# Bucketed attention with two gated layers: epsilon summed as a second column, two exponents in a burst step, normalisation behind the burst

## The reference, cut to what matters

```python
batch, n_heads, seq, head_dim = 2, 8, 768, 64
q_bits = (einsum('bhsd,dk->bhsk', q, proj) > 0)        # 6 bits, the same for k
mask = q_bucket[:, :, :, None] == k_bucket[:, :, None, :]
scores = where(mask, scale * q @ k.T, -1e9)
attn = exp(scores - max(scores))
attn = attn / (sum(attn, axis=-1) + 1e-09)
x = (attn @ v)  as (B, S, H * D)
gate = sigmoid(causal 5-tap convolution of x, per channel)
x = (gate * (x @ w_val)) @ w_out
xk, xr = x mixed with the row before it by mu_k, mu_r
out = sigmoid(xr @ w_r) * (relu(xk @ w_k) ** 2 @ w_v)
```

## Time and profile before

| | |
|---|---|
| median of 3 runs | 528.86 us (528.14 to 529.12) |
| the profiled execution's own time | 530.34 us |
| its span, first to last instruction | 528.5 us |
| TensorE matmul busy | 479.9 us, 91% |
| VectorE busy | 355.8 us, 67% |
| ScalarE busy | 281.0 us, 53% |
| GpSimd busy | 271.9 us, 51% |
| mean granted TensorE clock | 0.99 |

### The profile page before, as it was taken

How to read it: one execution, slowest core, us unless ns; L and a number is a source line. 1 busy time by engine, 2 the same in 40 slices (tenths; PEclk the granted TensorE clock), 3 DMA queues, 4 the chain that set the end, 5 groups by cost and what they waited for, 6 DMA issues and landing times.

```text
span 528.5 us, 9376 instructions
## 1 busy us (share of the span) xinstructions
PE 479.9 (91%) x3504; PEld 406.6 (77%) x3504; DVE 355.8 (67%) x603; ACT 281.0 (53%) x601; POOL 271.9 (51%) x259
## 2 busy tenths in 40 slices
PE   2879889898797888987999999999999999999997
PEld 1656666565565665665666999899999999999997
DVE  2676677976877869768785788778478578534211
ACT  3686775767558665776656453345245245144140
POOL 5592653826617458165505654646446446444240
PEclk9999999999899998999999999999999999999999
DMA  5021030210212102101013100100100100100101
GB/s 190 30 81 47 2 125 15 96 45 2 96 44 93 34 16 95 45 23 44 17 25 115 36 2 1 42 1 1 41 1 1 42 1 1 42 1 1 41 2 40
DMA packets 10574, 20.81 MB, mean 39 GB/s; under 512 B 1696, under 2 KB 6816, under 8 KB 10528
## 3 DMA queue, kind: packets, MB, share of 16 engines
q1 hardware_dynamic: 10224, 19.94, 11.5%
q10 hardware_dynamic: 304, 0.27, 0.2%
HBM read 17.06 MB, written 3.15 MB: 38 GB/s over the span
## 4 chain that ended last, share of the span: by engine, by line
PE 69%; DVE 15%; issue 8%; ACT 7%; DMA 1%; POOL 0%; ACTq 0%; DVEq 0%
PE ps L670 25%; PE ps L678 11%; PE ps L658 11%; PE ps L620 10%; PE ps L634 8%; DVE gate L828 3%; ACT q L434 2%; ACT probs L442 2%; DVE sums_e L805 2%; DVE negmax L786 2%; PE ps L644 1%; PE ps L595 1%; DVE pt L793 1%; DVE k L778 1%; DVE tmp_a L897 1%
## 5 line engine op out<-in xcount | busy, mean ns | idle before, releaser
L786 DVE TENSOR_REDUCE negmax<-ps 128x1 f32<-128x768 f32 x96 | 91.8, 956 | 62.9 <-PE ps L620 62.2
L620 PE MATMUL ps<-k,q 128*128 128x384 f32 x384 | 96.1, 374 | 20.5 <-ACT probs L442 18.4
L620 PEld LDWEIGHTS ps<-k,q 128*128 128x128 f32 x384 | 66.2, 197 | 37.4 <-issue 28.0
L634 PE MATMUL ps<-ident,probs 128*128 128x128 f32 x576 | 84.6, 282 | 10.8 <-DVE pt L793 10.3
L442 ACT ACTIVATE probs<-ps,negmax 128x768 f32<-128x768 f32 x96 | 86.5, 901 | 12.6 <-DVE negmax L786 10.6
L634 PEld LDWEIGHTS ps<-ident,probs 128*128 128x128 f32 x576 | 70.0, 145 | 19.9 <-DVE pt L793 11.5
L658 PE MATMUL ps<-pt,vals 128*64 128x384 f32 x384 | 70.2, 502 | 2.7 <-DVE x L818 2.7
L450 ACT ACTIVATE pt<-ps 128x384 f32<-128x384 f32 x96 | 46.7, 487 | 34.4 <-PE ps L634 33.1
L400 POOL TENSOR_TENSOR h_lo<-tmp_b,h_hi 128x256 fp32r<-128x256 f32 x48 | 38.7, 810 | 45.9 <-ACT h_hi L537 45.9
L828 DVE SCALAR_TENSOR_TENSOR gate<-x,conv_sb,gate 128x256 f32<-128x256 f32 x96 | 55.7, 580 | 2.5
L793 DVE COPY pt<-ps 128x384 f32<-128x384 f32 x96 | 52.2, 543 | 4.2 <-PE ps L634 3.9
(11 more groups left out here) (85 smaller groups left out, 1151.4 us busy)
## 6 DMA issues: line engine op xcount, KB each, us to landing
w_raw<-w SPq DMA_DIRECT2D x8, 640.0 KB, 4.2
raw_q<-qT SPq DMA_DIRECT2D x8, 384.0 KB, 3.0
raw_k<-kT SPq DMA_DIRECT2D x8, 384.0 KB, 4.7
vals<-v SPq DMA_DIRECT2D x16, 192.0 KB, 2.3
out<-w_raw SPq DMA_DIRECT2D x24, 128.0 KB, 1.7
w_raw<-w SPq DMA_DIRECT2D x4, 512.0 KB, 3.4
codes_f<-codes ACTq DMA_DIRECT2D x1, 256.0 KB, 5.5
proj_bd<-proj ACTq DMA_DIRECT2D x2, 1.5 KB, 4.2
```

Source lines behind the costliest of these rows:

```text
L620: last = pe.matmul(ps[:, 2 * par + half, 0:HALF], qq[h][:, q], kk[h][:, half * HALF:(half + 1) * HALF], start=first, stop=not first)
L634: last = pe.transpose(tbank[u][:, k * P:(k + 1) * P], probs[g % 2][:, kt * P:(kt + 1) * P], ident[:, :])
L786: dve.tensor_reduce(negmax[:, t:t + 1], score[g % 2], AX.XY, ALU.max, negate=True).then_inc(max_done, 1)
```

## The change

- `sums` has two columns for each tile. The exponent's sum goes into the first, the second is filled with 1e-9 once, and `add_eps` sums the two with a `tensor_reduce` in place of adding a constant.
- In a burst step g (from g = 8 on) ScalarE makes the exponent of tile g+2 directly behind the first-half copy of g, and leaves it out in the next step.
- VectorE's `normalise` moves from steps 2 and 8, where it took the head before the last, to steps 5 and 11 of a pair, for the head whose second burst that step issues. It stands behind the second-half copy and the hot keys and ahead of the taps. `normalise(14)` so leaves the hand-over and stands in front of the last epsilon.
- Taps: pairs 1 to 6 make two in step 8 and four in step 11, none in step 5; pair 7 makes two in step 5 and two in step 8.
- GpSimd's last `widen_reciprocals` moves ahead of `gates(1)` and `w2_low(0)`.

```diff
@@ def conv_taps(i, t)
     if i == PAIRS - 1:
-        return {5: range(34, 38), 8: range(38, 40)}.get(t, ())
+        return {5: range(36, 38), 8: range(38, 40)}.get(t, ())
+    if i and t == 8:
+        return range(6 * (i - 1), 6 * (i - 1) + 2)
     if i and t == 11:
-        return range(6 * (i - 1), 6 * (i - 1) + 4)
-    if i > 1 and t == 5:
-        return range(6 * (i - 1) - 2, 6 * (i - 1))
+        return range(6 * (i - 1) + 2, 6 * i)
     return ()
...
+def product_step(g):
+
+    return g >= KT and g % KT in PV_STEPS
...
-        sums = sb("sums", [P, TILES], F32, att)
+
+        sums = sb("sums", [P, TILES, 2], F32, att)
...
-        two_up = sem("two_up")
+        two_up, eps_up = sem("two_up"), sem("eps_up")
...
             gates(0)
+            widen_reciprocals(NHEADS - 1)
             gates(1)
             w2_low(0)
-            widen_reciprocals(NHEADS - 1)
             w2_low(1)
...
-                               accum_out=sums[:, t:t + 1]).then_inc(exp_done, 1)
+                               accum_out=sums[:, t, 0:1]).then_inc(exp_done, 1)
...
-                if g + 1 < PAIRS * TILES:
+
+                if g + 1 < PAIRS * TILES and not product_step(g - 1):
                     exp_tile(g + 1)
                 first_half_up(g)
+                if g + 2 < PAIRS * TILES and product_step(g):
+                    exp_tile(g + 2)
                 if tt == R_STEP and head:
                     reciprocals_up(head - 1)
...
             def add_eps(head):
                 cols = slice(head % 2 * KT, head % 2 * KT + KT)
+                dve.wait_ge(eps_up, 1)
                 dve.wait_ge(exp_done, KT * (head + 1))
-                dve.tensor_scalar(sums_e[:, :], sums[:, cols], 1e-9, None, ALU.add).then_inc(dve_sum, 1)
+                dve.tensor_reduce(sums_e[:, :], sums[:, cols, :], AX.X, ALU.add).then_inc(dve_sum, 1)
...
+            dve.memset(sums[:, :, 1:2], 1e-9).then_inc(eps_up, 1)
...
                 if tt == 0 and head:
                     add_eps(head - 1)
-                if tt == R_STEP and head >= 2:
-                    normalise(head - 2)
                 if g + 2 < PAIRS * TILES:
                     tile_max(g + 2)
...
+                if tt == KT - 1 and head:
+                    normalise(head - 1)
                 for n in conv_taps(i, t):
...
             y_low(1)
-            normalise(NHEADS - 2)
             gated(0, 2)
```

## The result

| | before | after |
|---|---|---|
| median of the runs timed together | 528.92 us (6 runs, 527.58 to 529.77) | 533.34 us (6 runs, 531.32 to 534.58) |
| profiled execution, own time | 530.34 | 533.01 |
| its span | 528.5 | 531.2 |

The ratio is 1.0084, with a 95% interval of 1.0061 to 1.0106: the changed kernel is slower by 4.4 us. The forecast was 533.4.

The account below looks back on a forecast made before the run. TensorE was taken to bound the kernel, holding 69% of the chain of waits. Terms -4.5 -11.9 +0.7 +12.6 +5.0 -0.6 +0.8 +2.5 = +4.6 us gave 533.4 against the median 528.86 (chance 0.45), range 526.0 to 537.5.

Parts of the forecast that it names:

- The exponents: Steps 2 and 8: step 2's exponent 0.75 us sooner, 4.5 in six pairs; pair 0 gains 1.04 in step 8.
- Step 5 loses its taps: Pairs 2 to 6: without step 5's taps, step 7's stall and its low clock go; 11.9 us saved.
- Epsilon: Epsilon add as a reduce: takes 0.19 us with its gap and adds nothing to the sum.
- Step 8: Two taps in step 8 wait beside GpSimd: 0.12 us lost a pair, 0.7 in six, instead of gaining 1.04.
- Step 11: Normalisation then four taps behind the burst: projection late, costing 2.14 us a pair, 1.86 in pair 6, 12.6 in all.
- The clock: Behind step 11's new idle of 2.1 us: low clock in three of six pairs, about 1.65 each, +5.0 us (0 to +9.9).
- Hand-over: From attention to the dense layers: late normalisation 14 makes TensorE's next layer start at 294.9 instead of 292.4, +2.5 us.
- Rival (1): Step 8: both taps run free of GpSimd, 1.16 us times six off, 526.4 us, faster; chance 0.15.
- Rival (2): Behind step 11's stall the clock stays up: 5.0 us off, 528.4 us, no change; chance 0.15.
- (3): The hand-over finds its place: 531.1 us; chance 0.15.
- (5): Epsilon swap fails: the reduce waits for GpSimd as the add did, 1.5 us a pair, 542 us; chance 0.03.
- Rival (4): Step 11's taps are covered by exponents in hand, only the first copy waits: 12.6 and 5.0 go, 515.8 us; chance 0.07.

Follow-up runs that it names:

- the two parts: The kernel before with the two moved exponents and the epsilon reduce, without the moved normalisation and taps: 506.26 us, ratio 0.9578.
- taps-first kernel: The changed kernel with the taps ahead of the normalisation instead of behind it, same taps in the same steps: 521.44 us, ratio 0.9863.
- the kernels of 505 to 507 us: The kernel before with exponents and reduce: 506.26 us; that with step 5's taps in step 2: 507.52; or with normalisation 14 ahead of y's low parts: 505.34.

## Why the prediction was right

The time came within 0.1 us of the forecast's 533.4, and the sign, the place of the new wait and its mechanism held. That the number is so close is luck: in the loop the sum was 3.4 us too high, and behind it 1.5 too low. Point by point:

- **The exponents.** Step 5's burst was to come 0.75 us sooner behind step 2's; it came 0.80 sooner. Pair 0's part was 0.6, and is 0.6 counted from its first burst; another 0.2 lies in front of that burst. "Nothing moves" in step 5 was wrong: step 8's burst follows step 5's by 7.87 us where it was 7.72, 0.9 in six pairs. It is the moved exponent that costs this, for the kernels with the exponents alone (pairs 1 and 2) and with the two parts have the same 7.86 or 7.87 with the old normalisation, and the one with the reduce alone has 7.73.
- **Step 5 loses its taps.** The wait of 2 us in step 7 is gone, and the pairs' lengths fell as forecast. But I gave the 11.9 us to the taps, and the experiments show that either of the other two parts does it: with the exponents alone all but 0.5 us of the stall is gone although the taps stay, with the reduce alone all but 0.1. The move could bring nothing here that they had not brought. The normalisation in step 5 costs nothing, as I said: step 7 waits 0.31 us for the copy, and then only 0.49 for the exponent where the two-parts kernel waits 0.68.
- **Epsilon.** I gave the swap nothing, as the taps' leaving takes the add out of GpSimd's way. The old add in the changed kernel confirms the nothing (533.82), not the reason, as the moved exponents take the add out of the way too. All sixteen reduces took 0.156 to 0.169 us.
- **Step 8.** I had both taps wait, the first for the cast. The first did not (0.38 us); the second did (2.00 us), and ended at d+4.26 instead of d+4.6. Step 11's burst follows at d+7.88, not d+8.25: a gain of 0.25 a pair instead of a loss of 0.12, 2.2 us in six pairs. The lost turn itself was right; with the clock this was the worst-sized term.
- **Step 11.** B+9.59 to the next burst was forecast, 9.63 measured; the wait 2.14, measured 2.07. The taps-first kernel shows the cause: with the taps in front the wait is 0.65.
- **The clock.** Three low stretches in the loop were taken, two came in the profiled execution (pairs 4 and 6); that of pair 4 cost 1.65 us (35.16 against 33.5), that of pair 6 about 1.3 (an estimate: 10.21 us from step 11's burst to the next, against 7.44 in the taps-first kernel and the 1.42 by which the two kernels differ in undisturbed pairs). That is 2.9 for a forecast 5.0. Which wait is followed by one is not decided by its length: pair 5's, the longest at 2.33 us, was not. One more low stretch came where I had none, behind the hand-over's wait of 3.74 us, and cost 1.6.
- **Hand-over.** Start at 13.35 behind the burst was forecast, 13.25 measured, with the turns beside GpSimd as worked out. One sign of being right, that the layer starts after 294, failed for the loop's sake: it starts at 293.53, as the burst before it came 1.3 us sooner.

Between the profiled executions the kernels differ by 2.7 us, not 4.6: in the loop I was 3.4 us too high (step 8 by 2.2 and the clock by 2.1, less 0.9 in step 5; the rest is small), from the hand-over on 1.5 too low (the low clock behind it). The medians differ by 4.4, since the profiled execution of before happened to be 1.4 over its median and that of after 0.3 under. Rival (1), that the taps of step 8 run free, did not happen; its size was fair, for moving them away brought 6.0 us where it had 7.0. Rival (2) is out by the low stretches in pairs 4 and 6, (3) by the 13.25, (5) by the sixteen reduces. Rival (4), that step 11's taps are covered, is ruled out by the taps-first kernel. What I had not weighed is how much the two good parts were worth by themselves: 22.7 us together. The forecast gave the exponents 4.5 and pair 0's 1.04, the reduce nothing, and put the 11.9 of step 7's stall down to the taps. A sum over the whole change does not show this, as each term counts only once whichever part brings it.

## What to carry to other kernels

An instruction that waits for a burst belongs behind all work that does not: in a strict queue, everything behind the waiting instruction is moved out of the burst's shadow with it, and the price is most of that work's length (here 1.4 us a pair for 1.8 us of taps). Measure each part of a change alone before judging it: here two parts bring 22.7 us and the third takes 27, and the sum looked like a small loss. And where two engines take turns on something, look at which of them starts first and by how much; here a start 0.1 to 0.2 us behind GpSimd's or 0.7 ahead of it decided 8 us.

## What the runs showed of the hardware

- A VectorE add of 128x6 elements that takes 0.17 us took 1.79 when GpSimd's subtraction had started 0.1 to 0.2 us before (five times in the kernel before), and 0.80 at most when it had not (there, with the exponents alone, and with the old add in the changed kernel). A reduce of 128x12 took 0.148 to 0.169 in every place of the nine kernels that have it. The add's small size did not shield it; the reduce's kind did.
- In the reverse order GpSimd waits: its subtraction of 1.82 us took 1.90 in the changed kernel's pair 2 and 1.99 to 2.00 in pairs 3 to 6 of the kernel before. There it started up to 0.2 us before a tap had ended, and lost about as much.
- TensorE's granted clock fell from 1.00 (2.4 GHz) to 0.50 (1.2 GHz) behind idle of 2.20 and 2.07 us in an otherwise dense stream, in pairs 4 and 6 of the changed kernel, and stayed there for some 3.4 us. It did not fall behind the same wait in pairs 1, 2, 3 and 5 (2.07, 2.07, 2.08 and 2.33 us). With waits of 0.9 us or less in pairs 1 to 6, as in the kernels of 505 to 507 us, the mean clock of the profiled execution was 1.00, and the runs of such a kernel lay within 1.4 us of each other, where those of the changed kernel lay 3.3 apart.
